# A causal convolution and two gated layers on one core: the first 24 slots with the gate in PSUM over four banks, the first two convolutions shared out anew, and weights rounded in half chunks

## What is computed

```python
x = softmax_taps_convolution(x, weight)    # (2, 4096, 192), causal, 7 taps, one set of taps for each of 8 heads
h = x @ w_in                               # 192 -> 2048
g = where(h >= 1, h, where(h <= -1, 0.0, (h + 1)**2 / 4))
x = g @ w_out                              # 2048 -> 192
h = x @ w_in2
g = h * sigmoid(1.702 * h)
out = g @ w_out2
```

## Time and profile before

| | us |
|---|---|
| median of three runs | 1263.33 |
| the profiled execution | 1260.91 |
| its span | 1259.1 |
| PE busy | 1217.3 |
| DVE busy | 881.0 |
| ACT busy | 760.6 |
| POOL busy | 477.5 |

### The profile page before, as it was taken

One profiled execution on the slowest core, in us unless ns is written; L12 is line 12 of the kernel. 1 busy time (PEld: TensorE's weight loads), 2 busy tenths in 40 slices (PEclk: granted clock), 3 DMA queues, 4 the chain that ended last, 5 costly groups with the idle time before them and its releaser, 6 DMA issues.

```text
span 1259.1 us, 17753 instructions
## 1 busy us (share of the span) xinstructions
PE 1217.3 (97%) x5918; PEld 1024.4 (81%) x5918; DVE 881.0 (70%) x1235; ACT 760.6 (60%) x1544; POOL 477.5 (38%) x416
## 2 busy tenths in 40 slices
PE   4979899999999999999999999999999999999998
PEld 2657778888888888888888888888888888888887
DVE  6876677768686776868677686777768686665633
ACT  3655666565756657565665757566575665755454
POOL 4959655327080441707145080623509063000000
PEclk7988999999999999999999999999999999999999
DMA  5320000000000000000000000000000000000000
GB/s 137 102 90 1 32 32 13 32 13 31 0 12 31 12 31 12 31 0 12 31 12 31 12 25 6 12 31 12 31 12 1 30 12 1 14 1 1 13 14 13
DMA packets 10656, 29.79 MB, mean 24 GB/s; under 512 B 1028, under 2 KB 5378, under 8 KB 10624
## 3 DMA queue, kind: packets, MB, share of 16 engines
q1 hardware_dynamic: 10624, 29.38, 7.3%
HBM read 23.09 MB, written 6.29 MB: 23 GB/s over the span
## 4 chain that ended last, share of the span: by engine, by line
PE 87%; POOL 5%; DVE 4%; ACT 2%; issue 2%; DMA 1%; SPq 0%; DVEq 0%; POOLq 0%; ACTq 0%
PE acc L483 15%; PE h L413 9%; PE h L414 9%; PE h L415 9%; PE h L416 9%; PE h L417 9%; PE acc L484 7%; PE acc L467 4%; PE acc L462 4%; PE acc L465 4%; PE acc L468 4%; PE acc L461 4%; POOL x_conv L357 2%; POOL prod L350 2%; DVE gate L676 1%
## 5 line engine op out<-in xcount | busy, mean ns | idle before, releaser
L541 ACT ACTIVATE clip<-clip,half 128x512 f32<-128x512 f32 x256 | 185.3, 724 | 397.9 <-DVE clip L669 397.7
L483 PE MATMUL acc<-w_down,g_hi 128*128 128x384 f32 x1024 | 306.5, 354 | 0.9 <-DVE g_lo L688 0.9
L676 DVE TENSOR_TENSOR gate<-h,clip 128x512 f32<-128x512 f32 x256 | 176.8, 691 | 145.4 <-ACT clip L541 137.2
L688 DVE TENSOR_TENSOR g_lo<-gate,g_hi 128x512 fp32r<-128x512 f32 x256 | 208.1, 813 | 89.0 <-ACT gate L557 84.6
L669 DVE TENSOR_SCALAR clip<-h 128x512 f32<-128x512 f32 x256 | 175.5, 686 | 116.8 <-PE h L417 116.6
L484 PE MATMUL acc<-w_down,g_lo 128*128 128x192 f32 x1024 | 256.6, 251 | 0.0
L682 DVE TENSOR_TENSOR g_lo<-gate,g_hi 128x512 fp32r<-128x512 f32 x256 | 242.0, 945 | 2.7 <-ACT g_hi L547 0.7
L350 POOL TENSOR_TENSOR x_conv<-x_in,tap_w 128x384 f32<-128x384 f32 (+2 forms) x30 | 26.6, 908 | 539.7 <-ACT raw L595 531.5
L357 POOL TENSOR_TENSOR x_conv<-x_conv,prod 128x384 f32<-128x384 f32 (+2 forms) x180 | 211.1, 1192 | 1.3
L350 POOL TENSOR_TENSOR prod<-x_in,tap_w 128x384 f32<-128x384 f32 (+2 forms) x180 | 208.1, 1180 | 4.9
L483 PEld LDWEIGHTS acc<-w_down,g_hi 128*128 128x128 f32 x1024 | 192.2, 188 | 14.3 <-issue 1.6
(11 more groups left out here) (120 smaller groups left out, 1958.2 us busy)
## 6 DMA issues: line engine op xcount, KB each, us to landing
x_in<-in_x SPq DMA_DIRECT2D x14, 960.0 KB
raw<-in_moe_w_out SPq DMA_DIRECT2D x8, 384.0 KB, 4.9
out_y<-y_out_a SPq DMA_DIRECT2D x8, 384.0 KB, 2.3
out_y<-y_out_b SPq DMA_DIRECT2D x7, 384.0 KB, 2.3
raw<-in_moe_w_in SPq DMA_DIRECT2D x4, 512.0 KB, 4.6
raw<-in_moe_w_in SPq DMA_DIRECT2D x8, 256.0 KB, 4.5
x_in<-in_x SPq DMA_DIRECT2D x1, 768.0 KB
x_in<-in_x SPq DMA_DIRECT2D x2, 283.5 KB
```

Source lines behind the costliest of these rows:

```text
L483: nc.tensor.matmul(acc2[j][:, 0:2 * D], hi[:, tok], w[:, 0:2 * D], start=first, stop=False)
L541: nc.scalar.activation(c, c, ACT.Square, bias=half[:, :], scale=0.5).then_inc(square_ready, 1)
L676: nc.vector.tensor_tensor(gate1[step.s % 2][:, :], bank1(step)[:, :], clip[step.s % 2][:, :], ALU.max).then_inc(gate1_ready, 1)
L688: nc.vector.tensor_tensor(g2_lo[k][:, :], gate2[:, :], g2_hi[k][:, :].bitcast(FP32), ALU.subtract).then_inc(g2_lo_ready, 1)
```

## The change

It touches the program up to slot 32, where the loop over tiles begins; the code of the loop and of the tail does the same as before. Steps 0 to 23 use four banks (`h0`, `h1`, `acc2_0`, `acc2_1`), the gate is written back into the step's own bank, and `up1` waits for the residue of the step four before. From slot 18 on `up1` runs one step further ahead. Tile 0's convolution begins with the last tap, which needs no rows of the neighbour partition, on all three engines; DVE uses one instruction a tap for its three heads and adds all six heads' products. Tile 1's convolution is shared: ACT makes the products of three heads in slots 4 to 12, POOL does five heads and adds ACT's. ACT rounds chunks in half pieces between `square` and `round_gate1`. Six chunks are loaded at the start (two into the idle `y_out` tiles). Chunks 12 to 15 come after the convolution of tile 2 in POOL's queue. PE's warm-up matmuls are tied to DVE's taps.

```diff
+    SOLO_BANKS = 4
+    AHEAD_FROM = F_TILES + SOLO_LAG
-    WARM_UP = 7
+    WARM_UP = 6
...
+        solo_banks = [h[0], h[1], acc2[0], acc2[1]]
...
         def bank1(step):
-            if isinstance(step.n, int) and step.n < BEHIND:
-                return h[step.n % 2]
-            return h[0]
+            return solo_banks[step.n % SOLO_BANKS] if alone1(step) else h[0]
+
+        def gate1_of(step):
+
+            return bank1(step) if alone1(step) else gate1[step.s % 2]
...
+        RAW_ORDER = [[0, 6, 10], [1, 7, 11], [4, 8, 12, 14], [5, 9, 13, 15]]
+        STAGED = [2, 3]
...
-            for n in range(RAW_RING):
+            for n in range(6):
                 load_raw(n)
 
             sp.wait_ge(xT_ready, 1)
             load_first(1)
-            for n in range(RAW_RING, 2 * N_CHUNKS):
+            for n in range(6, 12):
                 load_raw(n)
             for side in range(2):
                 sp.sem_inc(y_out_free[side], 16)
             load(2)
+            for n in range(12, 14):
+                load_raw(n)
             load(3)
+            for n in range(14, 2 * N_CHUNKS):
+                load_raw(n)
...
+            multiply(0)
+            multiply(1)
+            add(1)
+            split_weights(5)
+            for k in range(2, TAPS):
+                multiply(k)
+                add(k)
+                add_second(k - 1)
+                if k in (3, 4):
+                    split_weights(k + 3)
+            add_second(TAPS - 1)
+            for n in range(N_CHUNKS, 12):
                 split_weights(n)
+
+            pool.wait_ge(xT_ready, 2)
+            pool.wait_ge(x_loaded, 48)
+            convolve(2, slabs=2)
+            for n in range(12, 2 * N_CHUNKS):
                 split_weights(n)
...
-                if is_solo(step.tile, step.s):
-                    if step.n >= 2:
-                        pe.wait_ge(gate1_ready, step.n - 1)
+                if isinstance(step.n, int) and step.n <= BEHIND:
+
+                    if step.n >= SOLO_BANKS:
+                        pe.wait_ge(g1_lo_ready, step.n - SOLO_BANKS + 1)
...
+                ahead = solo and one.n >= AHEAD_FROM
+                if one is not None and not (ahead and one.n > AHEAD_FROM):
                     up1(one)
+                if ahead and one.n + 1 < BEHIND:
+                    up1(back(tile, side, s, -1))
...
+            for k in range(WARM_UP + TAPS - 1):
+                if k >= WARM_UP:
+                    pe.wait_ge(conv_dve, k - WARM_UP + 1)
+                nc.tensor.matmul(h[1][:, :], ident[:, :], gate2[:, :], start=True, stop=True)
...
+            pe.wait_ge(wp_ready, 2 * N_CHUNKS - DVE_CHUNKS)
             with nc.Fori(0, LOOP_PAIRS, engines=(pe.engine,), hint_back_edge=True) as i:
...
-            SPLIT_SLOTS = [{1: 4, 2: 5, 3: 6, 4: 7, 9: 8, 10: 9, 11: 10, 12: 11}, {0: 12, 3: 13, 4: 14, 5: 15}]
+            SPLIT_SLOTS = {0: [(4, 0)], 1: [(4, 1)], 2: [(5, 0)], 3: [(5, 1)], 8: [(6, 0), (6, 1)], 10: [(7, 0), (7, 1)],
+                           13: [(8, 0)], 15: [(8, 1)], 16: [(9, 0)], 18: [(9, 1)], 19: [(10, 0), (10, 1)],
+                           20: [(11, 0), (11, 1)], 22: [(12, 0)], 23: [(12, 1)], 24: [(13, 0)], 25: [(13, 1)],
+                           28: [(14, 0), (14, 1)], 29: [(15, 0), (15, 1)]}
+            SECOND_SLOTS = {4: 0, 5: 1, 6: 2, 7: 3, 9: 4, 11: 5, 12: 6}
```

More of the change, by code:

```diff
@@ L106, in conv_mlp_mlp @@
         raw_loaded = [sem(f"raw_loaded{k}") for k in range(RAW_RING)]
+        staged = [sem(f"staged{k}") for k in range(2)]
         w_hi_ready = sem("w_hi_ready")
@@ L336, in _, with conv_ops @@
             tap = tap_w[:, :].rearrange("p (h k) -> p h k", k=TAPS)
-            def convolve(tile, heads=HEADS, slabs=SLABS_PER_TILE, some=range(TAPS)):
+            def conv_ops(tile, heads=HEADS, slabs=SLABS_PER_TILE, last_tap_first=False):
                 base = tile * CONV_STEPS
@@ L358, in add, with convolve @@
                     ins.then_inc(conv_step, 1)
-                for k in some:
-                    if k > 2:
-                        pool.wait_ge(conv_step, base + 2 * k - 2)
+                return multiply, add
+            def convolve(tile, slabs):
+                multiply, add = conv_ops(tile, slabs=slabs)
+                for k in range(TAPS):
                     multiply(k)
@@ L478, in down2 @@
                 pe.wait_ge(g2_lo_ready, step.n + 1)
+                if isinstance(step.n, int) and step.n == 0:
+                    pe.wait_ge(g1_lo_ready, BEHIND)
+                    pe.wait_ge(x_from_dve, 4)
                 for j in range(SLABS_PER_TILE):
@@ L668, in clipped @@
                 dve.wait_ge(h1_ready, step.n + 1)
+                if alone1(step) and step.n >= 2:
+                    dve.wait_ge(gate1_ready, step.n - 1)
                 nc.vector.tensor_scalar(clip[step.s % 2][:, :], bank1(step)[:, :], -1.0, 1.0, ALU.max, ALU.min
@@ new lines, in multiply @@
+            def multiply(k):
+                at = TAPS - 1 - k
+                w = tap[:, HEADS - DVE_HEADS:HEADS, at:at + 1].unsqueeze(1).to_broadcast(shape)
+                dst = x_conv if k == 0 else prod[k % 2]
+                if k > 2:
+                    dve.wait_ge(conv_sum, k - 2)
+                nc.vector.tensor_tensor(by_head(dst[:, :, dve_cols]),
+                                        by_head(x_in[:, at:at + SLABS_PER_TILE, dve_cols]), w, ALU.mult
+                                        ).then_inc(conv_dve, 1)
@@ L818, in _ @@
+                nc.vector.tensor_tensor(o, o, prod[k % 2][:, :, sum_cols], ALU.add).then_inc(conv_sum, 1)
+            dve.wait_ge(x_loaded, 16)
+            dve.wait_ge(tap_step, 6)
+            multiply(0)
+            dve.wait_ge(x_halo, 16 * BATCH)
+            dve.wait_ge(x_zeroed, BATCH)
+            multiply(1)
+            for k in range(2, TAPS):
+                multiply(k)
+                add_products(k - 1)
             add_products(TAPS - 1)
@@ L821, in _ @@
             take_x(0, acc1)
-            for n in range(DVE_CHUNKS):
-                split_weights(n, 1)
+            split_weights(0, 1)
             run_head(slot)
```

260 lines of the change are left out of this document (172 added, 88 removed).

## The result

The changed kernel takes 1243.43 us in the median (1241.02 to 1243.94, 4 runs), beside 1262.98 for the kernel before (4 runs): ratio 0.9838 (95%: 0.982 to 0.9857), 19.6 us less. 1246 (1239 to 1254) was forecast. The profiled execution took 1242.95 us (span 1241.0), 17.96 less than the one of before.

The account below looks back on a forecast made before the run. POOL's queue was taken to bound the late stalls: tile 2's convolution ends at 109.0, plus 17.5 to tile 3, plus 33.2, puts slot 37 at 159.7 instead of 177.23. 17.5 less gives 1246 us (1239 to 1254).

Parts of the forecast that it names:

- Part 1: Tile 0's convolution: ends at 22.0 instead of 23.5; bounds 18.1 without contention, 24.7 if engines block each other for whole operations.
- Part 2: From tile 0's convolution to step 0: 3.7 us if the clock holds, first clip at 25.8; otherwise 1.5 us more.
- Part 3: Slots 0 to 13: DVE and ACT's loop 2.15 to 2.35 us, hidden by PE's 2.33; step 4 starts at 32.3.
- late case: POOL's chunk 4 starts before DVE's half of chunk 1, which waits: step 4 at 34.8, tile 1's end at 62.1.
- Part 4: POOL's queue up to tile 1's end: taken as 60.5, with PE waiting about 3 us at slot 14.
- Part 5: Tile 1's end to tile 2's convolution: 20.6 us, start at 81.1, 27.9 us long, end C at 109.0.
- Part 6: Given back behind tile 2: ACT waits 3 us for chunk 14's load in slot 28; tile 3 starts 17.5 after C.
- The sum: Slot 37 at 109.0 + 17.5 + 33.2 = 159.7 instead of 177.23; median 1263.3 - 17.5 = 1245.8, or 1246.
- the same pace from there: Sign to look for: the stretch from slot 37 to the end takes the same time as before.
- Less is gained: Rival, 0.20: blocking in tile 0 (+2.7), clock ahead of step 0 (+1.5), clock at slot 14 (+1.4), late case (+1.6): gain 10, 1253.
- Frees nothing: Rival, 0.06: residues still wait for POOL despite the gate in PSUM, solo slots stay near 3.2 us: gain 8, 1255.
- Slower: Rival, 0.03: ACT's wait for chunk 14 in slot 28 lasts 17.5 us longer than counted, the load taking 22 us.

Follow-up runs that it names:

- order undone: Changed kernel with chunks 12 to 15 back ahead of tile 2's convolution in POOL's queue and SP's loads, ACT rounding them in slots 21 to 26: 1261.06 us.
- chunks staged: Changed kernel with chunks 14 and 15 loaded into the two idle output tiles, ahead of chunks 12 and 13: 1239.83 us.
- the best version: Changed kernel with chunks 14 and 15 in idle output tiles, DVE's half of chunk 1 first, tile 2's taps between chunks 8 to 11: 1233.58 us.
- DVE first: Changed kernel with one wait more: POOL's chunk 4 starts only after DVE's second half of chunk 1: 1241.75 us.
- gate in SBUF: Changed kernel with the solo slots' gate back in two SBUF tiles, tile 1's products in two tiles of their own: 1252.45 us.
- old convolution: Changed kernel with tile 0's convolution as before: all heads behind the halo, one DVE instruction per head and tap: 1244.73 us.
- halo: Changed kernel with the first tap of tile 0 waiting for the halo rows on all three engines: 1243.79 us.
- whole chunks: Changed kernel with ACT rounding chunks 4 to 15 whole instead of in halves: 1240.71 us.

## Why the prediction was right, and where its steps were off

**What bounds.** Right, and the best supported: the time goes by POOL's queue. In the changed kernel, with the order undone and with chunks staged, tile 3's start and slot 37 move together (128.19 and 161.39; 147.36 and 180.56; 124.98 and 158.16) with 33.2 between them each time; in the best version, where PE no longer waits there, it is 35.4.

**Part 1, tile 0's convolution.** Forecast 22.0, measured 21.4, but for the wrong reason. The step that failed is the comparison with the old end: that was late through chunk 2's split, not through the shares of the heads. A tap took 1.76 us (forecast 1.87): DVE's product 0.73 and its sum of 576 columns 1.07, POOL's add of 192 columns 1.10 instead of the 0.61 that it takes with the old shares. The Trainium skill, page "SBUF — State Buffer", section "SBUF: two separate sides", would have the one engine wait for the other's whole instruction; the row of 2.91 us agrees, while tile 0 ended 3.3 us ahead of the 24.7 that this makes of the shares.

**Part 2, the way to step 0.** The clock did not hold. The warm-ups behind DVE's taps left PE idle for 3.25 us ahead of the transposes, these ran 0.21 us apart, and the first clip was at 26.94, not 25.8. With doubled warm-ups the clock was high in both kernels that have them, and the clip came 0.7 earlier. The wait makes the low clock likely and not certain: of the eight profiled kernels with single warm-ups and this wait, seven had it in the transposes and the one with DVE first did not.

**Part 3.** Its late case came, and slot 4 was at 35.90 (34.8 forecast for that case), 1.1 late by part 2. The two experiments that let DVE go first removed the 2.2 us by opposite means, a wait added and halves taken away. The loop of 2.33 is as forecast.

**Part 4.** Tile 1 ended at 63.01, 60.5 forecast, with the late case at 62.1. PE waited 2.58 there (3 forecast), and the low clock behind it came as in the rival.

**Part 5.** From tile 1's end to tile 2's start took 22.5 us instead of 20.6, of which some 1.5 is the clock (where it held, in the staged kernel, POOL waited 5.6 us for chunk 8 and not 7.2). The convolution took 27.0, forecast 27.9.

**Part 6.** Over-counted: 15.7 us from C, the end of tile 2's convolution, to tile 3 instead of 17.5. The load of chunk 14 was waited for 1.65 and not 3. With staging tiles 1.8 of it went; so this step's remedy was worth what the load cost.

**The sum.** Slot 37 was at 161.39, 159.7 forecast: the terms ahead of tile 2's end were together 3.5 late, the give-back 1.8 less. The time was nevertheless 2.4 lower than the sum's 1245.8, by two terms that have nothing to do with its mechanism. The part "the same pace from there" was wrong by 2.1 us. 1.5 of that is the gap on PE near 1048 of the kernel before, and for the other 0.6 there is no cause on record: 0.3 of it is there 51 us behind slot 37, the rest comes in small pieces. And the forecast laid 2.4 us on the profiled time, because the median of the kernel before was that far above its profiled execution; in the changed kernel it is 0.5, so 1.9 too much. With slot 37 right, and these two as forecast, the sum would have been 1247.5. That 1243.43 lies so near 1246 is in part luck.

**The rivals.** "Less is gained" was right in three of its four mechanisms (+1.1 for the clock ahead of step 0, +1.6 for the clock in slot 14, and the late case), yet the gain was 19.6 and not 10, as the fourth (blocking in tile 0) did not come and the give-back and the tail were smaller. "Frees nothing" is refuted by the residues and by the experiment with the gate in SBUF. "Slower" had no sign: the load was waited for 1.65 us.

## What to carry to other kernels

Find the queue whose order sets the late stalls, and count a faster stage only as far as that queue starts earlier: here fast solo slots were worth nothing where the queue held tile 2 behind chunks tied to later slots, and with the slow residues the whole change gained some 8 us less. Where two engines take turns at a resource, half a microsecond decides which goes first and 2.2 us follow; force the short operation that others wait for to go first. Read the profile of an undone part even if its time comes out as expected: tile 0's old convolution gave the forecast time by three terms that I had not counted.

## What the runs showed that I had not expected

The clock behind a short wait of PE. Eight profiled changed kernels have a wait of 2.1 us ahead of slot 37. In six of them it was followed by seven or eight matmuls at 0.6 us each (1.2 GHz), in the changed and the staged kernel by none. From slot 37 to the end the profiled executions took 1083.2 to 1083.3 us in five of the six (gate in SBUF, DVE first, halo, warm-ups doubled, order undone), 1085.0 in the sixth (old convolution), which has PE's gap of 1.53 besides, and 1081.6 in the two where it held. The same holds for the 2.6 us ahead of slot 14: from tile 1's transposes to the `down1` that waits for `y_part` it is 12.8 us in the four kernels in which the clock held (staged, halo, warm-ups doubled, old convolution) and 14.3 to 14.4 in the others (15.3 with the gate in SBUF), so it costs some 1.5 us. PE's matmuls behind slot 37 with doubled warm-ups show the moment:

```profile
159.79 0.60 PE L505 MATMUL h<-x_rest_a,rest_hi 128*128 128x512 f32 x1
160.19 0.63 PE L506 MATMUL h<-x_rest_a,rest_lo 128*128 128x512 f32 x1
```

What decides it is open. A gain ahead of such a wait can be lost behind it: 2.7 us in slot 37 came to 1.7 us in the median with DVE first, 2.4 to 1.2 with doubled warm-ups, and 0.9 to a loss of 0.4 with the tap waiting for the halo; with whole chunks, where the clock held, 2.6 came to 2.7.

Gaps without a visible cause. Near the loop's end and in the tail every profiled kernel has an engine that stands for 1 to 3.5 us at "issue": on PE itself before (1.5 and 1.7 in two executions), on DVE with 1.53 us passed on to PE in the kernel with the old convolution, and elsewhere on ACT or DVE (1.1 to 2.0 us) where PE does not wait for them. The gap on DVE lies at nearly the same place in all of them, 966.6 to 969.0 us behind slot 37 (959.0 with the gate in SBUF), the kernel before included; only with the old convolution did it reach PE, and only the kernel before has one on PE itself. One that PE feels moves a comparison by 1.5 us, more than half of what is taken here for a measurable difference. Its cause is open; no run tried to move it.
